# Attention scores over 128 contraction rows, rough scores over 96, the maximum's row at 96, and head 1 rounded directly behind head 0

## The reference

```python
scores = scale * np.matmul(q, k.transpose(0, 1, 3, 2))
cum = np.cumsum(np.maximum(s, 0.0), axis=-1)
bias = -(cum[:, :, :, None] - cum[:, :, None, :])
scores = np.where(causal, -1000000000.0, scores + np.minimum(bias, 0.0))
scores = scores - np.max(scores, axis=-1, keepdims=True)
attn = np.exp(scores)
attn = attn / (np.sum(attn, axis=-1, keepdims=True) + 1e-09)
return np.matmul(attn, v).astype(np.float32)
```

## Time and profile before

| | us |
|---|---|
| median of 3 runs | 1340.58 |
| lowest, highest | 1340.01, 1343.24 |
| the profiled execution's own time | 1338.8 |
| its span, first to last instruction | 1336.9 |
| PE busy | 1295.5 (97%) |
| PEld busy | 1153.6 (86%) |
| DVE, ACT, POOL busy | 486.7, 363.6, 147.6 |

### The profile page before, as it was taken

The page is one execution under the profiler, slowest core; times in us unless marked ns, Lnnn a source line. Parts: engine busy times, 40 slices in busy tenths (PEclk is TensorE's granted clock), DMA queues, the critical chain, the costliest instruction groups (busy, mean ns, idle before and its releaser), DMA issues.

```text
span 1336.9 us, 17458 instructions
## 1 busy us (share of the span) xinstructions
PE 1295.5 (97%) x6613; PEld 1153.6 (86%) x6613; DVE 486.7 (36%) x1092; ACT 363.6 (27%) x682; POOL 147.6 (11%) x222
## 2 busy tenths in 40 slices
PE   8999994899999996999999999999999999999999
PEld 5888893888888885899999999999999999999998
DVE  5333325755555454144323323323323323323321
ACT  4333332444444432212212212212212212212211
POOL 5433441111111044100000000000000000000000
PEclk8555557899999997999999999999999999999999
DMA  6334206344444452301101101101101101100000
GB/s 141 96 95 95 60 1 221 106 178 173 176 173 178 178 177 77 127 1 63 64 1 63 63 0 63 63 0 63 63 0 63 63 0 63 63 0 0 24 24 24
DMA packets 24757, 102.90 MB, mean 77 GB/s; under 512 B 5440, under 2 KB 10048, under 8 KB 20752
## 3 DMA queue, kind: packets, MB, share of 16 engines
q1 hardware_dynamic: 18288, 85.89, 19.2%
q0 software_dynamic: 3360, 11.01, 2.8%
q10 hardware_dynamic: 3072, 5.51, 1.2%
HBM read 87.68 MB, written 10.22 MB: 73 GB/s over the span
## 4 chain that ended last, share of the span: by engine, by line
PE 94%; DVE 2%; DMA 1%; issue 1%; ACT 1%; POOL 0%; POOLq 0%; DVEq 0%
PE bank L701 13%; PE bank L700 13%; PE bank L699 13%; PE bank L681 13%; PE bank L682 13%; PE bank L683 13%; PE bank L631 6%; PE bank L614 2%; PE bank L580 2%; PE bank L615 2%; PE bank L637 1%; PE bank L733 1%; PE bank L594 1%; PE bank L645 1%; DMA x_sb<-x_dram,gather_at 1%
## 5 line engine op out<-in xcount | busy, mean ns | idle before, releaser
L681 PE MATMUL bank<-xTh,w1h 128*128 128x384 f32 (+1 forms) x1024 | 344.5, 336 | 3.0 <-DVE xTl L1138 1.6
L682 PE MATMUL bank<-xTl,w1h 128*128 128x384 f32 (+1 forms) x1024 | 342.4, 334 | 0.0
L683 PE MATMUL bank<-xTh,w1l 128*128 128x384 f32 (+1 forms) x1024 | 341.7, 334 | 0.0
L936 ACT ACTIVATE hh<-bank 128x384 fp32r<-128x384 f32 (+1 forms) x256 | 123.5, 482 | 658.0 <-PE bank L683 655.3
L701 PE MATMUL bank<-w2h,hl 128*128 128x512 f32 (+1 forms) x768 | 302.4, 394 | 0.0
L700 PE MATMUL bank<-w2l,hh 128*128 128x512 f32 (+1 forms) x768 | 300.7, 392 | 0.0
L699 PE MATMUL bank<-w2h,hh 128*128 128x512 f32 (+1 forms) x768 | 299.8, 390 | 0.0
L1158 DVE SCALAR_TENSOR_TENSOR hl<-bank,hh 128x384 fp32r<-128x384 f32 (+1 forms) x256 | 139.5, 545 | 371.1 <-ACT hh L936 367.7
L681 PEld LDWEIGHTS bank<-xTh,w1h 128*128 128x128 f32 x1024 | 193.9, 189 | 5.5 <-issue 2.1
L682 PEld LDWEIGHTS bank<-xTl,w1h 128*128 128x128 f32 x1024 | 193.9, 189 | 1.2
L683 PEld LDWEIGHTS bank<-xTh,w1l 128*128 128x128 f32 x1024 | 193.9, 189 | 0.0
(11 more groups left out here) (171 smaller groups left out, 761.3 us busy)
## 6 DMA issues: line engine op xcount, KB each, us to landing
raw<-in_w SPq DMA_DIRECT2D x15, 2048.0 KB, 8.0
raw<-in_w1b SPq DMA_DIRECT2D x8, 2048.0 KB, 7.7
raw<-in_w2b SPq DMA_DIRECT2D x8, 2048.0 KB, 7.7
k_raw<-in_kT SPq DMA_DIRECT2D x16, 288.0 KB, 5.9
y_dram<-x_sb ACTq DMA_DIRECT2D x16, 256.0 KB
q_raw<-in_qT SPq DMA_DIRECT2D x8, 288.0 KB, 5.8
q_two<-w2l SPq DMA_DIRECT2D x8, 288.0 KB, 3.3
x_dram<-x_sb SPq DMA_DIRECT2D x1, 2304.0 KB, 9.4
```

Source lines behind the costliest of these rows:

```text
L681: pe.matmul(dst, w1h[:, c, fs], xTh[:, c, ts], start=(c == 0), stop=False)
L682: pe.matmul(dst, w1h[:, c, fs], xTl[:, c, ts], start=False, stop=False)
L683: mm = pe.matmul(dst, w1l[:, c, fs], xTh[:, c, ts], start=False, stop=(c == DC - 1))
L936: act.activation(hh[:, f, 0:n_cols], bank[:, f % UP_BANKS, 0:n_cols], ACT.Relu).then_inc(st.hh_ready, 1)
```

## The change

The extra rows of `q_top` and `k_top` now reach to partition 127. In `q_top` they are cleared to zero first, then rows 64 and 65 are set to one; the maximum goes to row 96, and a zero to row 97. In `k_top` they are all one but for the two rows of the sum. The rough scores contract over rows 0 to 95, the scores over all 128. The tile of maxima has two columns in place of four. There are six warm-up matmuls in place of nine. ScalarE rounds k and q of head 1 directly behind those of head 0, ahead of its loop, and its loop begins at step -13 and leaves heads 0 and 1 out of its own rounding.

```diff
-        AUG = HD + 4
+        ROWS_ROUGH = HD + 32
...
-        q_top = [w2l_flat[0:AUG, i * N:(i + 1) * N] for i in range(HEADS_RING)]
-        k_top_all = sb("k_top", [AUG, HEADS_RING, N], F32R, where=attn)
+        q_top = [w2l_flat[:, i * N:(i + 1) * N] for i in range(HEADS_RING)]
+        k_top_all = sb("k_top", [P, HEADS_RING, N], F32R, where=attn)
...
-        aug = sb("aug", [P, MAX_RING, STEPS, 4], F32R, where=attn)
+        aug = sb("aug", [P, MAX_RING, STEPS, 2], F32R, where=attn)
...
-        WARM_UPS = 9
+        WARM_UPS = 6
...
-                    sp.wait_ge(aug_ready, 3 + h)
+                    sp.wait_ge(aug_ready, 2 + h)
...
-            pool.memset(aug[:, :, :, 0:3].bitcast(F32), 1.0).then_inc(aug_ready, 1)
-            pool.memset(aug[:, :, :, 3:4].bitcast(F32), 0.0).then_inc(aug_ready, 1)
+            pool.memset(aug[:].bitcast(F32), 0.0).then_inc(aug_ready, 1)
...
-                pool.memset(k_top[w][HD:AUG, :].bitcast(F32), 1.0).then_inc(aug_ready, 1)
+                pool.memset(k_top[w][HD:P, :].bitcast(F32), 1.0).then_inc(aug_ready, 1)
...
-                q = q_top[w][0:HD + 2, b * S + t * P:b * S + t * P + rows]
+                q = q_top[w][0:ROWS_ROUGH, b * S + t * P:b * S + t * P + rows]
...
-                    mm = pe.matmul(bank[0:rows, first + c0 // BANK, 0:c1 - c0], q, k_top[w][0:HD + 2, b * S + c0:b * S + c1],
+                    mm = pe.matmul(bank[0:rows, first + c0 // BANK, 0:c1 - c0], q, k_top[w][0:ROWS_ROUGH, b * S + c0:b * S + c1],
...
-                    mm = pe.matmul(bank[0:4, MAX_AT, at:at + rows], aug[0:rows, n % MAX_RING, t, :], ident_r[0:rows, 0:rows],
+                    mm = pe.matmul(bank[0:2, MAX_AT, at:at + rows], aug[0:rows, n % MAX_RING, t, :], ident_r[0:rows, 0:rows],
...
-                act.copy(q_top[w][HD:AUG, b * S + i0:b * S + i1], bank[0:4, MAX_AT, 0:i1 - i0]).then_inc(max_placed, 1)
+                act.copy(q_top[w][ROWS_ROUGH:ROWS_ROUGH + 2, b * S + i0:b * S + i1], bank[0:2, MAX_AT, 0:i1 - i0]).then_inc(max_placed, 1)
...
             high_q(0)
             high_k(0)
-
-            for k in range(-K_HIGH_AHEAD + 2, ALL):
+            high_k(1)
+            high_q(1)
+
+            for k in range(-ROUGH_AHEAD, ALL):
                 kh, qh = high_at(k)
-                if kh is not None:
+                if kh is not None and kh > 1:
...
-                if qh is not None:
+                if qh is not None and qh > 1:
...
             def q_rows(w):
-                v.memset(q_top[w][HD:AUG, :].bitcast(F32), 1.0).then_inc(q_rows_ready, 1)
+                v.memset(q_top[w][HD:P, :].bitcast(F32), 0.0).then_inc(q_rows_clear, 1)
+                v.wait_ge(q_rows_clear, w + 1)
+                v.memset(q_top[w][HD:HD + 2, :].bitcast(F32), 1.0).then_inc(q_rows_ready, 1)
...
-                                       accum_out=aug[0:rows, n % MAX_RING, t, 2:3]).then_inc(max_ready, 1)
+                                       accum_out=aug[0:rows, n % MAX_RING, t, 0:1]).then_inc(max_ready, 1)
```

More of the change, by code:

```diff
@@ L152, in build @@
         ident_rounded = sem("ident_rounded")
+        q_rows_clear = sem("q_rows_clear")
         q_rows_ready = sem("q_rows_ready")
@@ L454, in _ @@
             pool.wait_ge(const_ready, 6)
-            pool.wait_ge(aug_ready, 2)
             for w in range(HEADS_RING):
-                pool.memset(k_top[w][HD:AUG, :].bitcast(F32), 1.0).then_inc(aug_ready, 1)
-            pool.wait_ge(aug_ready, HEADS_RING + 2)
+                pool.memset(k_top[w][HD:P, :].bitcast(F32), 1.0).then_inc(aug_ready, 1)
+            pool.wait_ge(aug_ready, HEADS_RING + 1)
             def low_part(h, c, k):
@@ L1062, in _ @@
             v.wait_ge(const_ready, 6)
-            v.wait_ge(aug_ready, 2)
+            v.wait_ge(aug_ready, 1)
             link(v.tensor_copy(rinv[:].rearrange("p a b -> p (a b)"), ones[:, 0:2 * STEPS]))
```

## The result

The changed kernel takes 1300.82 us, the median of four runs (1288.66, 1295.73, 1305.9, 1328.61); the kernel before, beside it, 1340.3 (1339.12 to 1343.24). The ratio is 0.967, with a 95% interval of 0.959 to 0.976; it leaves out the run of 1328.61 as a slow one, though its distance to the others is part of the effect, as will be seen. The forecast was 1279, between 1256 and 1344. So the change is faster, by 39.5 us and not by 62, and where runs of the kernel before lie within some 4 us, these lie 40 us apart. The profiled execution is the one of 1305.9.

A forecast was written before the change was run, and what follows sets the result against it. Attention was taken as bound by TensorE at half its clock. Terms -64.5 (clock), +4 (GpSimd), -2.7 (stretch to 201.5), +1.3 (memset) gave -61.9: 1276.9 us for the execution, 1279 for the median, range 1256 to 1344.

The forecast's parts named there:

- case A: Attention's first half: wider matmul rows raise TensorE's clock; 1279 us, own range 1256 to 1320, chance 0.50.
- rows 3 and 4: Profile groups: low-clock stretch includes matmuls over 66 and 68 rows; every matmul ahead of the clock's rise uses 128.
- Case C: Attention: the added rows do nothing to the clock, only the added memset remains; 1342 us, chance 0.29.
- one head later, at 47: Attention: clock falls near 24 us, rises at 47, leaving 149 us, 6.45 heads, for -64.5 us.
- Case B: Attention: clock rises late or is lost again at a head's wait for k; 1323 us, chance 0.11.
- the sign named for A: Attention: a granted clock of 1.00 in most slices would show the forecast right.
- The head at the high clock: Each attention head: 23.12 us halved to 11.56 plus 1.5 wait, so 13.1 (11.6 to 15.8), gaining 10.0.
- The bias sum: Start, VectorE: the second memset delays the sum and SP's issues down to the doubled k; +1.3 us (0 to 2.1).
- a term that the text had put at nothing: Start: VectorE's first row maximum, 2.1 us late at 15.16, hidden by TensorE's 2.18 us wait before 22.45.
- Case D: Start: fewer warm-ups and later sum rows idle TensorE, so the start runs at low clock; 1348 us, chance 0.10.
- GpSimd's parts of the expert's weights: Last eight attention steps: eight weight parts, 10.2 us, formerly hidden beside slow steps; charged +4 us (0 to 6).
- ScalarE's early rounding: Start: rounding head 1 early delays head 0's maxima under the stall's cover; costed at nothing, about 1 us without it.

## Why the prediction was right, and where it was off

**Rows move the clock.** Right, in case A and in its reason, the contrast of rows 3 and 4: the rows alone give the rise, and the traces of 98 rows or of rough scores over 66 have none. Case C, that zeros count for nothing, is refuted by the same runs. The wider contraction costs nothing by itself, as the earlier trace rows had it: 774 and 793 ns for 512 columns, before and now, at the low clock. The Trainium skill's rule (TensorE: Matmul & The Clock Gate, Part 1) that busyness releases the throttle misses it again: in the changed kernel PE is busy 85.30 of 85.30 us at 0.50.

**When it rises, and whether it stays: the step that failed.** The text let the clock rise "one head later, at 47" and stay, 6.45 heads at 10.0. In the profiled run it rose at 21.8, was lost at 35.4, and rose again at 120.7 only. From there to 168 there are 47.3 / 13.86 = 3.4 heads, at 9.26 us each 31.6 of the 33.0 us that the span lost; the rest is put down to the high stretch at the start, less the low one ahead of it, without a working. Case B's mechanism, a head's wait that loses the clock, was held to be another outcome, at 0.11; it is part of this one. The text had both halves in hand: it charged each head 1.5 us for its wait, and it knew that a wait of 2.10 us had lost the clock. Yet in the sum a wait costs only its own length, and the clock stays high through all of them. The runs show idles of 0.83 to 1.64 us at heads of the changed kernel at the high clock, a fall behind the longest of them, and a clock that stays up once such idles are taken away (1260.86 us).

That the time lies within 1256 to 1344 tells little, since this range reaches from A to beyond C; and the sign named for A, 1.00 in most slices of the attention, came for about half of them. That it lies near A is in part luck: a head's gain of 9.26 where 10.0 was forecast, times a number of heads that was 3.4 in this run and, by the mean clocks, another in each of the others, which gained from 12 to 52 us.

The Trainium skill (TensorE: Matmul & The Clock Gate, "A second HAM failure mode: psum-queue depth-cycling") tells of a kernel in which small idles between groups of matmuls made the clock go back and forth; the traces agree, with falls behind idles of 1.00 to 2.58 us, though idles of 1.03, 1.05, 1.09 and 2.28 us elsewhere were passed.

**The head at the high clock.** 13.1 was forecast, 13.86 measured with the stall, 12.71 without. The 1.5 us taken for the wait is near the 1.15 between these two, of which 0.83 shows as an idle in the head measured.

**The start.** The bias sum was to move by 1.32; it did, from 3.52 (L1052) to 4.84 (L1055 now). SP's first sum row moved by 0.95 and the doubled k by 1.02, since that first step of the sum was itself 0.37 shorter. But head 1's first rough scores came at 24.49, 2.04 late where 1.3 was forecast, and with no idle time ahead of them: TensorE had run the first head's rough scores at 0.50, from 15.0 to 21.7. This comes from a term that the text had put at nothing: VectorE's first row maximum, late behind the added memsets, was held to be hidden. It came at 14.84 (15.16 was forecast, 13.09 before), TensorE stood idle for 2.19 us waiting for it, from 13.46 to 15.65, and in that time the clock fell. Case D had seen a low clock at the start, but from an idle ahead of the first rough matmul, for want of warm-ups; that idle was 1.20 us. The rows alone, with nine warm-ups and no such idle, have the same wait of 2.18 us and the low clock behind it, from 15.9 to 19.3, so the missing warm-ups are not needed for it. The clock returned, so that it only ate a little of the gain.

**GpSimd's parts of the expert's weights** were charged 4 us in the last steps. From 120.7 to 170 us TensorE waited for GpSimd by 0.4 us in all, so the term was too large.

**ScalarE's early rounding** was costed at nothing, under the cover of the stall, and at about 1 us without it. In the changed kernel no wait for it shows, with TensorE at the low clock there; where the start is made earlier the cover is gone, and it is the idle of 2.19 to 2.28 us above, behind which two traces lost the clock and a third did not.

## What to carry to other kernels

Where the granted clock is low over a stretch in which TensorE is always busy, look at the rows that its matmuls use, not only at its idle time: filling unused rows, with zeros in one operand, costs no time here and can be what brings the clock back. Then look for what loses it again: at double the pace, waits that were hidden appear, and one idle of about a us at a head cost more through the clock than by itself. A spread of tens of us between runs, where there was none before, together with the mean clock of each, was here the sign of a clock that is lost and regained at different moments; the version without those idles is both faster and steady, 1260.9 us within some 2.

## What was not expected

That runs of one kernel differ by 40 us on the clock alone. That an idle of 1.00 us lost the clock at one place and idles of 1.09 and even 2.28 us did not at others: what decides is not settled. Nor is it why, with all the rows, the clock came back at 97.6 us in one trace and at 145.6 in another, and where the quick runs at 1308 us with 66 rows had their high stretch. Whether 68 rows would hold the clock to the end without the last stall was not tried.
